# Folding the attention result by transposes and a VectorE reduction, with the scaling moved to Pool

## What is computed

```python
scores = scale * np.matmul(q, k.transpose(0, 1, 3, 2))
scores = np.where(mask, scores, -1000000000.0)   # mask: q and k have the same nearest centroid
attn = np.exp(scores - np.max(scores, axis=-1, keepdims=True))
attn = attn / (np.sum(attn, axis=-1, keepdims=True) + 1e-09)
x = np.matmul(attn, v)                           # then laid out as (batch, tokens, 512)
x = fourier_mix_and_mlp(x); return conv_gated_mlp(x)
```

## Time and profile before

| | us |
|---|---|
| median of 3 runs | 784.91 (783.96 to 788.56) |
| the profiled execution | 781.4 |
| its span | 779.6 |
| attention stage within it | about 25 to 301 |
| TensorE, VectorE, ScalarE, Pool busy | 729.7, 420.5, 300.0, 249.2 |

### The profile page before, as it was taken

One profiled execution on the slowest core, in us unless ns is written; L12 is line 12 of the kernel. 1 busy time (PEld: TensorE's weight loads), 2 busy tenths in 40 slices (PEclk: granted clock), 3 DMA queues, 4 the chain that ended last, 5 costly groups with the idle time before them and its releaser, 6 DMA issues.

```text
span 779.6 us, 10436 instructions
## 1 busy us (share of the span) xinstructions
PE 729.7 (94%) x4001; PEld 648.2 (83%) x4001; DVE 420.5 (54%) x722; ACT 300.0 (38%) x622; POOL 249.2 (32%) x236
## 2 busy tenths in 40 slices
PE   4799999989989998998999999999999989899998
PEld 4699898989988987997888888888888878898886
DVE  3688989888888878667311131113111168884310
ACT  2467667666767775121101111101101136453311
POOL 3456655646446623005720000000014035641000
PEclk9999999999999999999999999999999999999999
DMA  4434445232445303002310000001022051100011
GB/s 141 133 85 110 106 110 142 73 111 70 120 121 150 90 21 109 1 1 81 109 28 0 1 1 1 0 1 55 0 69 94 0 149 41 28 13 28 28 41 54
DMA packets 26865, 49.02 MB, mean 63 GB/s; under 512 B 4032, under 2 KB 11456, under 8 KB 26304
## 3 DMA queue, kind: packets, MB, share of 16 engines
q1 hardware_dynamic: 24368, 39.49, 17.9%
q0 software_dynamic: 2448, 8.87, 3.5%
HBM read 37.33 MB, written 3.15 MB: 52 GB/s over the span
## 4 chain that ended last, share of the span: by engine, by line
PE 73%; DVE 12%; ACT 5%; issue 3%; POOL 3%; DMA 2%; SPq 1%; ACTq 0%; POOLq 0%; DVEq 0%
PE ps L1162 23%; PE ps L1241 17%; PE ps L1320 9%; PE ps L1306 6%; PE ps L1090 5%; PE ps L1076 4%; PE ps L1033 3%; DVE pt_l L731 2%; PE ps L1064 2%; PE ps L1065 2%; ACT prob L536 2%; DVE row_min L724 2%; ACT pt_h L548 2%; DVE mask_n L765 1%; DVE gate L994 1%
## 5 line engine op out<-in xcount | busy, mean ns | idle before, releaser
L928 DVE SCALAR_TENSOR_TENSOR hid_l<-ps,hid_h 128x512 fp32r<-128x512 f32 x48 | 33.2, 691 | 203.3 <-ACT hid_h L632 203.3
L731 DVE TENSOR_TENSOR pt_l<-ps,pt_h 128x384 fp32r<-128x384 f32 x192 | 101.3, 550 | 37.7 <-ACT pt_h L548 37.3
L632 ACT ACTIVATE hid_h<-ps 128x512 fp32r<-128x512 f32 x48 | 28.7, 599 | 226.9 <-PE ps L1162 226.9
L548 ACT ACTIVATE pt_h<-ps 128x384 fp32r<-128x384 f32 x192 | 84.8, 491 | 68.3 <-PE ps L1076 67.6
L1076 PE MATMUL ps<-cst,prob 128*128 128x128 f32 x576 | 84.5, 282 | 15.2 <-ACT prob L536 9.8
L724 DVE TENSOR_REDUCE row_min<-ps 128x1 f32<-128x768 f32 x96 | 90.3, 941 | 11.2 <-PE ps L1065 11.2
L536 ACT ACTIVATE prob<-ps,row_min 128x768 f32<-128x768 f32 x96 | 87.0, 906 | 8.2 <-DVE row_min L724 7.9
L1076 PEld LDWEIGHTS ps<-cst,prob 128*128 128x128 f32 x576 | 65.8, 145 | 27.4 <-ACT prob L536 18.4
L1064 PE MATMUL ps<-k,q 80*128 80x384 f32 x192 | 74.6, 389 | 3.7 <-ACT prob L536 1.5
L1162 PE MATMUL ps<-un_h,w_h 128*128 128x512 f32 x192 | 75.7, 394 | 1.4 <-DVE un_l L922 1.4
L1241 PE MATMUL ps<-w_h,hid_h 128*128 128x512 f32 x192 | 76.0, 396 | 0.0
(11 more groups left out here) (131 smaller groups left out, 1546.5 us busy)
## 6 DMA issues: line engine op xcount, KB each, us to landing
stage<-in_moe_w_ch SPq DMA_DIRECT2D x16, 256.0 KB, 3.4
w_raw<-in_moe_w_ch SPq DMA_DIRECT2D x16, 256.0 KB, 2.6
raw_d<-in_q SPq DMA_DIRECT2D x8, 384.0 KB, 3.7
raw_d<-in_k SPq DMA_DIRECT2D x8, 384.0 KB, 5.6
raw_qk<-in_q SPq DMA_DIRECT2D x16, 192.0 KB, 3.2
raw_qk<-in_k SPq DMA_DIRECT2D x16, 192.0 KB, 3.4
raw_v<-in_v SPq DMA_DIRECT2D x16, 192.0 KB, 2.5
q<-q SPq DMA_DIRECT2D x16, 192.0 KB, 2.9
```

The costliest lines, as they stand in the source:

```text
L548: nc.scalar.activation(pt_h[a][:, R * hf:R * hf + R, (t % R) * P:(t % R + 1) * P], ps[:, 4 + hf, 0:HALF].rearrange("p (j c) -> p j c", j=R ...
L731: nc.vector.tensor_tensor(pt_l[a][part], ps[:, 4 + hf, 0:HALF].rearrange("p (j c) -> p j c", j=R), as_f32(pt_h[a][part]), ALU.subtract).th ...
```

## The change

- `fold_o` makes three transposes with `ident` in place of the three matmuls with `fold`; the constant `fold` is gone. Bank 6 then holds, for each tile, 64 columns of the high part's result and 64 of the low part's.
- VectorE's `join_o` adds the two by a `tensor_reduce` from bank 6 into a new SBUF tile `joined` and increments a new semaphore, o_joined, which `values` waits for in place of x_stored. `join_o(n, 1)` stands ahead of `minimum(m, 5)`.
- Pool's `store_x` multiplies `joined` with the reciprocals into x: half 1 of head n - 3 behind `scale_q(n + 1)` in pass n, half 0 of head n - 2 behind `split_v(n)`. The last head's are left to VectorE.
- As `joined` and `rden` have one buffer for each half, `invert(n, a)` and `join_o(n, a)` wait until half a of head n - 1 is stored.
- row_sum gets a second column that holds 1e-9, so the denominator is a `tensor_reduce` over two columns.

```diff
@@ Pool
             nc.gpsimd.memset(cen_b[:, :, :], 0.0).then_inc(cen_cleared, 1)
+            nc.gpsimd.memset(row_sum[:, :, 1], SUM_EPS).then_inc(eps_set, 1)
...
+            def store_x(n, a):
+                i, s = n // 2, n % 2
+                pool.wait_ge(rden_done, 2 * n + a + 1)
+                pool.wait_ge(o_joined, AHEAD + 2 * n + a + 1)
+                nc.gpsimd.tensor_tensor(x[:, s, R * a:R * a + R, i * D:(i + 1) * D], joined[:, a, :, :],
+                                        rden[:, a, :].unsqueeze(2).broadcast_to([P, R, D]),
+                                        ALU.mult).then_inc(x_stored, 1)
...
                 if n < NH - 1:
                     scale_q(n + 1)
+                if n >= 3:
+                    store_x(n - 3, 1)
                 split_w1(n)
                 split_v(n, n % 2)
+                if n >= 2:
+                    store_x(n - 2, 0)
...
+            store_x(NH - 3, 1)
+            store_x(NH - 2, 0)
+            store_x(NH - 2, 1)
             pool.wait_ge(x_stored, AHEAD + 2 * NH - 2)
@@ VectorE
             def denominator(n, s, a):
                 rows = slice(6 * s + R * a, 6 * s + R * a + R)
-                nc.vector.tensor_scalar(den[:, a, :], row_sum[:, rows], SUM_EPS, None,
-                                        ALU.add).then_inc(den_done, 1)
+                dve.wait_ge(eps_set, 1)
+                nc.vector.tensor_reduce(den[:, a, :], row_sum[:, rows, :], axis=AX.X,
+                                        op=ALU.add).then_inc(den_done, 1)
 
             def invert(n, a):
                 dve.wait_ge(den_done, 2 * n + a + 1)
+                if n:
+                    dve.wait_ge(x_stored, AHEAD + 2 * n + a - 1)
                 nc.vector.reciprocal(rden[:, a, :], den[:, a, :]).then_inc(rden_done, 1)
+
+            def join_o(n, a):
+                dve.wait_ge(fold_ready, AHEAD + 2 * n + a + 1)
+                if n:
+                    dve.wait_ge(x_stored, AHEAD + 2 * n + a - 1)
+                nc.vector.tensor_reduce(joined[:, a, :, :],
+                                        ps[:, 6, 0:HALF].rearrange("p (r l d) -> p r d l", r=R, l=2),
+                                        axis=AX.X, op=ALU.add).then_inc(o_joined, 1)
...
-                store_x(n, s, 0, i)
+                join_o(n, 0)
...
                 minimum(m, 1 - s, 4)
-                step(m, 1 - s, 3)
-                store_x(n, s, 1, i)
+                store_low(m, 3, 0)
+                store_low(m, 3, 1)
+                join_o(n, 1)
+                minimum(m, 1 - s, 5)
@@ TensorE
-                    if 2 * n + a:
-                        pe.wait_ge(x_stored, AHEAD + 2 * n + a)
+                    if not (isinstance(n, int) and 2 * n + a == 0):
+                        pe.wait_ge(o_joined, AHEAD + 2 * n + a)
...
                 for r in range(R):
-                    last = nc.tensor.matmul(ps[:, 6, r * D:(r + 1) * D], o_s[:, r * P:(r + 1) * P], fold,
-                                            start=True, stop=True)
+                    last = nc.tensor.transpose(ps[:, 6, r * P:(r + 1) * P], o_s[:, r * P:(r + 1) * P], ident)
```

More of the change, by code:

```diff
@@ L59, in sb @@
             return stack.enter_context(nc.sbuf_tensor(name, [P] + shape, dt))
-        cst = sb(main, "cst", [P + D + C])
+        cst = sb(main, "cst", [P + C])
         ident = cst[:, 0:P]
-        fold = cst[:, P:P + D]
-        first = cst[:, P + D:P + D + C]
+        first = cst[:, P:P + C]
         ln = sb(main, "ln", [B * NT, 11])
@@ L104, in build @@
         row_min = sb(att, "row_min", [2 * NT])
-        row_sum = sb(att, "row_sum", [2 * NT])
+        row_sum = sb(att, "row_sum", [2 * NT, 2])
+        joined = sb(att, "joined", [2, R, D])
         den = sb(att, "den", [2, R])
@@ L185, in build @@
         x_stored = sem("x_stored")
+        o_joined = sem("o_joined")
         mask_ready = sem("mask_ready")
@@ L190, in build @@
         den_done, rden_done = sem("den_done"), sem("rden_done")
+        eps_set = sem("eps_set")
         cen_dup, cen_built = sem("cen_dup"), sem("cen_built")
@@ L538, in exponent @@
                                      bias=row_min[:, col:col + 1], scale=-1.0,
-                                     accum_out=row_sum[:, col:col + 1]).then_inc(exp_ready, 1)
+                                     accum_out=row_sum[:, col, 0:1]).then_inc(exp_ready, 1)
             def store_high(n, t):
@@ L697, in _ @@
             dve.sem_inc(x_stored, AHEAD)
+            dve.sem_inc(o_joined, AHEAD)
             dve.wait_ge(cen_rooted, 1)
@@ L773, in denominator @@
                 rows = slice(6 * s + R * a, 6 * s + R * a + R)
-                nc.vector.tensor_scalar(den[:, a, :], row_sum[:, rows], SUM_EPS, None,
-                                        ALU.add).then_inc(den_done, 1)
+                dve.wait_ge(eps_set, 1)
+                nc.vector.tensor_reduce(den[:, a, :], row_sum[:, rows, :], axis=AX.X,
+                                        op=ALU.add).then_inc(den_done, 1)
             def invert(n, a):
                 dve.wait_ge(den_done, 2 * n + a + 1)
+                if n:
+                    dve.wait_ge(x_stored, AHEAD + 2 * n + a - 1)
                 nc.vector.reciprocal(rden[:, a, :], den[:, a, :]).then_inc(rden_done, 1)
+            def join_o(n, a):
[5 more added lines that the diff above has]
+                                        axis=AX.X, op=ALU.add).then_inc(o_joined, 1)
             def store_x(n, s, a, i):
                 dve.wait_ge(rden_done, 2 * n + a + 1)
-                dve.wait_ge(fold_ready, AHEAD + 2 * n + a + 1)
-                nc.vector.tensor_tensor(x[:, s, R * a:R * a + R, i * D:(i + 1) * D],
-                                        ps[:, 6, 0:R * D].rearrange("p (r d) -> p r d", r=R),
+                dve.wait_ge(o_joined, AHEAD + 2 * n + a + 1)
+                dve.wait_ge(x_stored, AHEAD + 2 * n + a)
+                nc.vector.tensor_tensor(x[:, s, R * a:R * a + R, i * D:(i + 1) * D], joined[:, a, :, :],
                                         rden[:, a, :].unsqueeze(2).broadcast_to([P, R, D]),
@@ L818, in head @@
                     denominator(n, s, 1)
+                    join_o(n, 0)
+                    invert(n, 1)
                     store_x(n, s, 0, i)
-                    invert(n, 1)
                     for m in range(2 * R):
                         pair_low_part(0, m)
+                    join_o(n, 1)
                     store_x(n, s, 1, i)
@@ L1416 @@
     add("chan_tab", channel_table())
-    two = np.concatenate([np.eye(D), np.eye(D)])
-    add("constants", np.concatenate([np.eye(P), two, np.tile(C - np.arange(C), (P, 1))], 1).astype(np.float32))
+    add("constants", np.concatenate([np.eye(P), np.tile(C - np.arange(C), (P, 1))], 1).astype(np.float32))
     args.append(nc.dram_tensor("out_0", (B, S, DM), F32, kind="ExternalOutput").ap())
```

## The result

The changed kernel takes 873.8 us (median of 4 runs, 872.3 to 875.2) against 784.4 for the kernel before (median of 4): a ratio of 1.1155, 95% interval 1.1115 to 1.1196. It is 11.6% slower, 89 us; 860.6 was forecast, within 835 to 880.

What follows compares the result with a forecast made beforehand. A plain attention step was taken as a closed round of TensorE turn, evacuation, exponential, turn. Summed loop lengths moved invert(14, 1) from 282.18 to 357.9 us, +75.7, so 784.9 became 860.6 us, range 835 to 880.

Steps and rivals of the forecast that it cites:

- the closed loop through Pool: Attention stage: invert(n, 1) waits for Pool's store behind raw_qk, Pool for values; 20.6 us per ordinary head, 16.7 before.
- The rival of throughput alone: Stores always in time; Pool's 1.36 us a head delays only the last heads by 4.1: 789 us, chance 0.03.
- the faster one: Stores in time and gains counting: VectorE's denominators some 4 us, TensorE's folds 3.0; 7 us less, 778, chance 0.04.
- that of a Pool running ahead: Values don't hold Pool, so its own round counts: 17.4 us a head, +53 us, 838, chance 0.07.
- invert(1, 1), from the start: VectorE's head 1 reciprocal, held until Pool's stores behind scale_q(4): at 75.0 us, a stall of 10.1.
- seven ordinary heads: Heads 2, 4, 5, 6, 8, 9, 12 of the attention stage: one loop of 20.6 us each.
- heads 3, 7, 11 (masks): SP loads raw_qk only behind masks made in the same head: loops of 24.8, 27.1 and 26.5, together 78.4 us.
- head 10 (dots): Pool waits for all dots before it queues the table's DMA: a loop of 31.1 us.
- from the reciprocal to the end of the values: Loop step from invert(n-1, 1) to the end of values(n-1, 1), when ScalarE stores o_s: 5.3 us.
- Two of the signs that I named: Attention stage: scores, turns and values keep their durations; reciprocals of half 1 start 20 to 21 us apart.
- The rival of a longer loop: Pool's store of 1 us adds 7, 6.4 for 5.3 up to values adds 8, mask waits more: above 880, chance 0.06.
- The rest of the loop: Pool from split_v(n+1) to scale_q(n+3), 13.0 us, then scale_q 0.9 and two stores 1.36.

Runs made afterwards that it cites:

- e1: The changed kernel with two buffers for the reciprocals, so invert(n, a) waits for the stores of head n-2: 789.6 us, ratio 1.0082 to the kernel before.
- e2: The changed kernel with Pool's store_x(n-3, 1) moved ahead of scale_q(n+1), so ahead of the wait for raw_qk: 795.7 us, ratio 1.0163 to the kernel before.
- e5: The changed kernel with three more copies of v's high part on Pool in each pass, 1.8 us in all: 889.0 us, ratio 1.1337.
- e3: The changed kernel with 11 unread fp32 matmuls on TensorE ahead of the scores of tile 3 in heads 2 to 13: 859.9 us, ratio 1.0979.
- e4: The kernel before with the stored constant alone, denominators as reductions over two columns: 780.4 us, ratio 0.9961.
- e7: The changed kernel with both cures, reciprocals in two buffers and store_x(n-3, 1) ahead of scale_q: 780.6 us, ratio 0.9964 to the kernel before.
- e8: e7 with Pool's wait for the last dots and both table DMAs moved behind pass 12: 777.1 us, ratio 0.9904 to the kernel before.

## Why the prediction was right, and what it lacked

**The mechanism: right, and shown.** The wait of invert(n, 1) for a store behind the wait for raw_qk, and the closed loop through Pool, were named; e1 and e2 take it away at either end, and e5 lengthens it. The rival of throughput alone (789) and the faster one (778) fell with the reciprocals, as said; that of a Pool running ahead fell with its 68 us of waiting for the values.

**The terms of the sum.** Intervals between the reciprocals of half 1 in us, computed and measured in the changed kernel:

| | computed | measured |
|---|---|---|
| invert(1, 1), from the start | 75.0 | 72.6 |
| seven ordinary heads | 7 x 20.6 = 144.2 | 158.4 (22.2 to 23.1 each) |
| heads 3, 7, 11 (masks) | 24.8, 27.1, 26.5 = 78.4 | 26.9, 25.5, 26.8 = 79.2 |
| head 10 (dots) | 31.1 | 30.7 |
| heads 13, 14 | 2 x 14.6 = 29.2 | 16.0, 14.6 = 30.7 |
| invert(14, 1) | 357.9 | 371.5 |

Of the 13.6 us that were missing the ordinary heads have 14.2; the others cancel nearly. The first interval was 2.4 us too long in the forecast, since Pool reached scale_q(4) at 71.19 us and not at 72.70 and took 1.4 us from there to the release, not 2.3; and head 13 took 16.0 for 14.6. In the ordinary heads one step of the loop was wrong: from the reciprocal to the end of the values, 5.3 computed. Over the seven of them, up to the split of v, it took 54.7 us for 37.1. In the turn shown above it took 152.02 - 144.07 = 7.95, because TensorE came out of the stall at 1.2 GHz. Before, its granted clock was 1.00 over the whole stage, and I priced its work at those durations, though I had just worked out that it would stand still for some microseconds in every head. Two of the signs that I named failed: turns and values did not keep their durations, and the ordinary reciprocals stood 22 to 23 us apart, not 20 to 21. The rival of a longer loop had this step in its list, at 6.4 us and without a reason; it was 7.8 in the mean. The rest of the loop was 13.0 + 0.68 = 13.7 by the forecast and 165.69 - 152.02 = 13.7 in this turn (93.9 over the seven, for 95.8), and from scale_q to the reciprocal 1.4 for 1.6. So 3 us too much in these two terms hid a part of the miss, 1.3 of it in the stores (505 ns measured, 600 taken). At full clock, in e3, the whole is 20.0 for 20.6: 5.5 for 5.3, 13.1 for 13.7 and 1.4 for 1.6. That the time came within 13 us is thus no proof that every term was right.

**The prices.** The groups of the attention stage in the changed kernel, as the earlier trace rows:

```profile
L1110 PEld LDWEIGHTS ps<-cst,prob 128*128 128x128 f32 x558 | 71.5, 156 | 35.1 <-ACT prob L554 21.5 <-issue 10.4
...
L807 DVE TENSOR_REDUCE joined<-ps 128x192 f32<-128x384 f32 x29 | 15.9, 547 | 0.0
...
L442 POOL TENSOR_TENSOR x<-joined,rden 128x192 f32<-128x192 f32 x29 | 14.6, 505 | 8.2 <-DVE joined L807 8.1
...
L1134 PEld LDWEIGHTS ps<-cst,o_s 128*128 128x128 f32 x88 | 11.5, 141 | 1.0
...
L794 DVE TENSOR_REDUCE den<-row_sum 128x3 f32<-128x6 f32 x30 | 4.4, 147 | 0.0
```

Pool's store takes 505 ns, the lower bound that I gave. The join was put at 542 ns and takes 547; the denominator at 0.16 us and takes 147 ns. The share of its gain that lies on the chain I estimated at 4 us; alone it gave 3, by its interval 0.5 to 5.6 (e4). The loads of the turns show the clock, 156 ns for 144.

**The fold.** Three loads of 141 ns for six of 191 are as read. What they are worth alone no run here shows; in e7 and e8 the sum of fold, join and offload isn't to be told from nothing.

**What lay behind.** From invert(14, 1) to the end 1.5 us more, put at nothing.

## What to carry to other kernels

When work is given to another engine, the buffer that it reads becomes a promise of that engine's queue: look up what stands ahead of the releasing instruction there, above all a wait for a DMA, and how that queue in turn is held by the one that waits. If the way leads back, each round costs the length of the whole loop, however idle the engines are; a second buffer of 24 bytes was worth 82 us of the 89 here, one changed place in the order 76. And price a forecast stall twice: once for its length, and once for what the stalled TensorE's clock costs behind it.

## What the runs showed of the hardware

- TensorE's clock was down behind eleven of the twelve stalls (granted 0.50 to 0.72 in the 5 to 6 us from the reciprocal on), and stayed at 1.00 behind the shortest, of 2.15 us. In the turn above it was idle from 141.8 to 145.7 us, ran at 0.50 to 0.52 until about 151, and loads that take 0.19 us took 0.33. Over the stage from 25 to 375 us it was granted 0.87. Matmuls that nobody reads, in part of the idle time, gave back 14 us of 874.
- A multiplication on VectorE with both inputs in SBUF took up to 1.78 us beside Pool's subtraction, where it took 0.36 us in the median; with one input in PSUM it took 0.34 to 0.35 us every time. A reduction of the row sums stayed at 148 ns where the addition of a constant took 584 in the mean.
